# A fused attention, MLP and routed-expert kernel: the opening and the first block in another order

## What is computed

```python
# 1. linear attention with a decaying state: 4 sequences, 8 heads, 768 tokens, head size 48
for t in range(S):
    kt, vt, rt = (k[:, :, t], v[:, :, t], r[:, :, t])
    cur = np.einsum('bhd,bhe->bhde', u[None] * kt, vt)
    y[:, :, t] = np.einsum('bhd,bhde->bhe', rt, state + cur)
    state = w[None, :, :, None] * state + np.einsum('bhd,bhe->bhde', kt, vt)
# 2. dense MLP on x = y as 3072 rows of 384: w_in 384x2048, w_out 2048x384
h = np.maximum(x @ w_in, 0.0); x2 = h * h @ w_out
# 3. eight experts (384 -> 1024 -> 384) of 384 tokens each; a greedy assignment by sorted logits
out[mask] = np.maximum(x2[mask] @ w1[e], 0.0) @ w2[e]
```

## Time and profile before

| | |
|---|---|
| time, median of 3 executions | 803.26 us (802.25 to 804.04) |
| the profiled execution | 805.37 us |
| its span in the trace | 803.3 us |
| TensorE matmul busy | 785.6 us, 98% |
| VectorE busy | 537.0 us, 67% |
| ScalarE busy | 273.4 us, 34% |
| GpSimd busy | 175.8 us, 22% |

### The profile page before, as it was taken

One profiled execution on the slowest core, in us unless ns is written; L12 is line 12 of the kernel. 1 busy time (PEld: TensorE's weight loads), 2 busy tenths in 40 slices (PEclk: granted clock), 3 DMA queues, 4 the chain that ended last, 5 costly groups with the idle time before them and its releaser, 6 DMA issues.

```text
span 803.3 us, 16845 instructions
## 1 busy us (share of the span) xinstructions
PE 785.6 (98%) x6663; PEld 654.2 (81%) x6663; DVE 537.0 (67%) x1280; ACT 273.4 (34%) x511; POOL 175.8 (22%) x169
## 2 busy tenths in 40 slices
PE   8799999999999999999999999989999999999996
PEld 5677777777777877777777888668999999999996
DVE  7887767776677776777776545665867757667321
ACT  3443324433433343334434444311222122122321
POOL 5523142212222222222120040001122221231211
PEclk9999999999999999999999999999999999999999
DMA  8734225666666666666675566327467466564950
GB/s 265 247 135 135 83 95 184 224 214 207 200 208 215 206 205 220 214 214 221 214 260 170 173 215 212 137 70 287 163 229 262 169 224 218 222 250 144 341 218 29
DMA packets 62910, 158.72 MB, mean 198 GB/s; under 512 B 8304, under 2 KB 11632, under 8 KB 62832
## 3 DMA queue, kind: packets, MB, share of 16 engines
q1 hardware_dynamic: 56880, 144.28, 53.2%
q0 software_dynamic: 3072, 9.44, 3.6%
q10 hardware_dynamic: 2880, 3.93, 1.3%
HBM read 106.24 MB, written 51.38 MB: 196 GB/s over the span
## 4 chain that ended last, share of the span: by engine, by line
PE 90%; DMA 4%; DVE 2%; issue 1%; SPq 1%; ACT 0%; POOL 0%; POOLq 0%; DVEq 0%
PE ACC L1534 25%; PE U L1508 24%; PE ACC L1727 13%; PE U L1714 13%; DMA stage<-in_dw 3%; PE P L1625 3%; PE P L1391 3%; PE P L1408 2%; PE P L1478 2%; PE P L1400 1%; PE ACC L1571 1%; PE P L1490 1%; DMA WL<-split_low 1%; PE P L1650 1%; PE P L1452 0%
## 5 line engine op out<-in xcount | busy, mean ns | idle before, releaser
L1010 DVE TENSOR_TENSOR hr<-hr 128x512 f32<-128x512 f32 x96 | 67.9, 707 | 80.9 <-ACT hr L774 80.7
L1508 PE MATMUL U<-XH,WH 128*128 128x512 f32 x285 | 113.4, 398 | 0.0
L1508 PE MATMUL U<-XH,WL 128*128 128x512 f32 x285 | 112.9, 396 | 0.0
L1508 PE MATMUL U<-XL,WH 128*128 128x512 f32 x285 | 112.9, 396 | 0.0
L774 ACT ACTIVATE hr<-U 128x512 f32<-128x512 f32 x96 | 57.3, 596 | 162.0 <-PE U L1508 160.0
L1534 PE MATMUL ACC<-HH,WH 128*128 128x512 f32 x252 | 105.6, 419 | 2.7 <-DVE HL L1024 2.7
L1534 PE MATMUL ACC<-HL,WH 128*128 128x512 f32 x252 | 99.9, 397 | 0.0
L1534 PE MATMUL ACC<-HH,WL 128*128 128x512 f32 x252 | 99.8, 396 | 0.0
L1040 DVE TENSOR_TENSOR stage<-stage 128x512 fp32r<-128x512 f32 x80 | 68.8, 861 | 26.2 <-ACT stage L754 23.9
L886 ACT ACTIVATE HH<-U 128x384 fp32r<-128x384 f32 x64 | 31.5, 492 | 145.3 <-PE U L1714 142.3
L754 ACT ACTIVATE HH<-hr 128x512 fp32r<-128x512 f32 x84 | 53.1, 632 | 77.2 <-DVE hr L1010 77.2
(11 more groups left out here) (252 smaller groups left out, 1472.2 us busy)
## 6 DMA issues: line engine op xcount, KB each, us to landing
stage<-in_ew SPq DMA_DIRECT2D x80, 256.0 KB, 3.6
split_high<-stage SPq DMA_DIRECT2D x80, 256.0 KB, 2.1
split_low<-stage SPq DMA_DIRECT2D x80, 256.0 KB, 2.5
WH<-split_high SPq DMA_DIRECT2D x40, 512.0 KB, 5.9
WL<-split_low SPq DMA_DIRECT2D x40, 512.0 KB, 6.6
tok<-in_tok SPq DMA_DIRECT2D x24, 640.0 KB, 7.0
rk<-in_rk SPq DMA_DIRECT2D x22, 448.0 KB, 5.8
stage<-in_dw SPq DMA_DIRECT2D x8, 768.0 KB, 7.8
```

The lines of the kernel that those rows point to most:

```text
L1010: tt(hr[:, s % 2, :], hr[:, s % 2, :], hr[:, s % 2, :], ALU.mult).then_inc(sq_done, 1)
L1508: ins = mm(U[s % 2][:, :], w_up((WH, WL)[a], k, s), (XH, XL)[b][:, q, k, :], start=(n == 0), stop=(n == 3 * KT - 1))
```

## The change

Nothing is computed in another way and no instruction is added or taken out; the order changes in five places.

1. DVE, opening: the low part XL of sequence 0 and the masks of sequence 2 stand ahead of the scaling of sequence 3.
2. SP, opening: chunk 1 of the weights is asked for right behind the transposed rows of unit 4, ahead of its token rows.
3. POOL, opening: both products of sequences 2 and 3 stand ahead of the weighted keys of sequence 2.
4. ACT and DVE: chunk 1 is split at the end of the opening, ahead of the relu and the square of the first hidden tile, and no longer behind them.
5. PE, first block: the down tile of step 2 moves behind the up tile of step 3; the down tile of step 3 moves to step 4, where two down tiles follow each other.

```diff
@@ sync
             def opening_unit(b):
-                sp.wait_ge(at_mm, 2 * b + 2)
                 sp.wait_ge(y_mm, b + 1)
                 sp.wait_ge(st_mm, b + 1)
-                load_unit(BATCH + b, b, b)
+                load_tok(BATCH + b, b)
 
             sp.wait_ge(ld_stage[0], 16)
-            opening_unit(0)
+            sp.wait_ge(at_mm, 2)
+            load_rk(BATCH, 0)
             sp.wait_ge(at_mm, 2 * BATCH)
             load_weights(1)
+            opening_unit(0)
+            load_rk(BATCH + 1, 1)
             opening_unit(1)
@@ gpsimd
             pool.wait_ge(scaled, 1)
-            for b in range(BATCH):
-                unit(0, b, False)
+            for b in range(2):
+                products(0, b, True)
+                weighted(0, b, False)
+            for b in range(2, BATCH):
+                products(0, b, False)
+            for b in range(2, BATCH):
+                weighted(0, b, False)
             pool.wait_ge(tab, TAB_STEPS)
             with pool.Fori(1, NC) as c:
                 for b in range(BATCH):
-                    unit(c, b, True)
+                    products(c, b, False)
+                    weighted(c, b, True)
@@ scalar, block
                         nc.scalar.activation(hr[:, s % 2, :], U[s % 2][:, :], ACT.Relu).then_inc(relu_done, 1)
-                        if not post and s == 0:
-                            split_chunk(1)
@@ scalar, opening
                 if b == 1:
                     split_chunk(0)
+            split_chunk(1)
 
             blocks(act, body)
@@ vector, block
-                    if moe and not post and s == 0:
-                        split_chunk(1)
@@ vector, opening
             diagonal(0, 1)
+            task(0, 0, opening_out(0), "Y", 0)
+            opening_mask(2)
             opening_scale(3)
-            opening_mask(2)
-            task(0, 0, opening_out(0), "Y", 0)
             diagonal(0, 2)
...
             scale(1, 0)
+            split_chunk(1)
@@ tensor
                     if post or s > 0:
                         up(m, 1 - q, s)
+                    if moe and not post and s == LAG + 1:
+                        pe.wait_ge(wlo_done, 2)
+                        down(m, 0)
                     for n, kind, b in tasks_at(s, att, moe, post):
                         task(c, (att, moe, post), n, kind, b)
-                    if moe and not post and s >= LAG and (s - LAG) % GROUP == 0:
+                    if moe and not post and s > LAG and (s - LAG) % GROUP == 0:
                         pe.wait_ge(wlo_done, 2 * ((s - LAG) // GROUP) + 2)
...
-                    elif moe and (s >= LAG or post):
+                    elif moe and not post and s == 2 * LAG:
+                        down(m, 1)
+                        down(m, LAG)
+                    elif post or s > 2 * LAG:
                         down(m if s >= LAG else m - 1, (s - LAG) % NF1)
```

More of the change, by code:

```diff
@@ L654, in by_head, with products @@
                 return t.rearrange("p (h d) -> p h d", d=HDIM)
-            def unit(c, b, state):
+            def products(c, b, first):
                 u = BATCH * c + b
@@ L661, in unit @@
                 nc.gpsimd.tensor_tensor(r_t, r_t, k_t, ALU.mult).then_inc(rk_step, 1)
-                if not state:
+                if first:
                     pool.wait_ge(ld_urow, 16)
@@ L665, in unit, with weighted @@
                 nc.gpsimd.tensor_tensor(r_t, r_t, urow[:, :], ALU.mult).then_inc(rku_done, 1)
+            def weighted(c, b, state):
+                u = BATCH * c + b
+                k_t = tok[:, b, DM:2 * DM]
                 if not state:
```

## The result

The changed kernel takes 806.25 us (median of 7 runs, 803.83 to 808.01), the kernel before, in 7 runs beside it, 802.25 (801.30 to 804.04). The ratio is 1.0046 with an interval of 1.0027 to 1.0065: **slower**, by some 0.5%, where 801.0 had been forecast. The profiled execution has 808.01 us and a span of 806.2.

The account below looks back on a forecast made before the run. TensorE's waiting and slow clock around the first down tile were taken as the bound. 2.35 us won, 0.1 taken off, gave 2.2: 805.37 to 803.1 profiled, median 803.26 to 801.0, range 799.4 to 801.6 (chance 0.55).

Parts of the forecast that it names:

- What bounds the kernel: First block: TensorE's 2.7 us wait ahead of the first down tile plus 1.6 us of slow clock, 4.3 us at most.
- The clock's 1.6 us: First down tile and the up tile behind it: time lost to a lowered clock after TensorE stood still, 1.6 us.
- The same 2.2 off it gives 801.0: Whole kernel: the 2.2 us gain taken from the median of 803.26 us gives 801.0 us.
- Opening, masks ahead of the scaling: Opening on VectorE: masks run inside the load wait, TensorE ends the opening about 1.4 us earlier; costed at nothing.
- Chunk 1 at 30.5, token rows at 32.8: Opening's transfers: the weight chunk lands at 30.5 us, unit 4's token rows take its old place at 32.8.
- The diagonal at 36.4, blocked: VectorE, unit 4: the diagonal waits for GpSimd's two products, slowed by mutual blocking, until 36.4 us.
- the unblocked 34.9: VectorE, unit 4: start of the diagonal if VectorE and GpSimd do not block each other, 34.9 us.
- Split of chunk 2 ends at 45.1, up tile 4 with it: First block: VectorE's split ends at 45.1 us, before 43.96; up tile 4 waits 0.5 to 1 us for it.
- From up tile 4 to up tile 5, 7.6 us: TensorE, first block: 5.5 us plus a down tile of 2.10; up tile 5 starts at 52.7, 2.35 us won.
- The clock: "I expect no fall": First block: the long wait is cut into about 1.5 and 0.5 us, so the clock stays up; 1.6 us within 2.35.
- B: Rival: unit 4's token rows land late, near 36 us, and clock is lost in the open; 805.2 us, chance 0.12.
- A: Rival: VectorE's train eats the gain, TensorE waits for chunk 2 until 46 or later; 802.6 us, chance 0.27.

Follow-up runs that it names:

- the second trace: The kernel before, run and traced once more with nothing changed: 802.11 us, span 800.3.
- experiment 8's second kernel: The kernel before with only 24 unused products added in TensorE's wait at the first gathers: 803.30 us, ratio 1.0003.
- experiment 9: Changed kernel with unit 4's high and low parts made early and 24 unused products at the gathers, 804.00 us, beside the same with the old opening, 802.03 us.
- experiment 3: The changed kernel with TensorE's old order, so the opening's changes alone on the kernel before: 805.80 us, ratio 1.0024.
- experiment 7's first kernel: The kernel before with only chunk 1 asked for ahead of the token rows and split early: 803.35 us, ratio 1.0001.
- experiment 7's second kernel: The kernel before with only the opening's new order of VectorE's masks and GpSimd's products: 803.87 us, ratio 1.0018.
- experiment 9's first trace: Trace of the changed kernel with unit 4's high and low parts made early and 24 unused products at the gathers: 804.00 us, ratio 1.0011.

## Why the prediction was wrong, step by step

*What bounds the kernel.* Right as a reading of one execution, wrong as a yardstick. The clock's 1.6 us and 1.1 us of the wait belonged to the profiled execution and not to every one: the second trace has neither. Nor is it rare: experiment 8's second kernel, which is before up to the gathers, had the wait of 2.7 us and the fall again. "The same 2.2 off it gives 801.0" took from the median what the median does not hold. The profiled execution lay 2.1 us above the median; that this might sit in just the place under study was the warning.

*Opening, masks ahead of the scaling: costed at nothing.* TensorE was earlier, and it was worth nothing, as said: in the part with masks and GpSimd alone the wait ahead of the down tile was 2.9 us against 1.6 in the second trace of before. VectorE gained 0.5 us only (split of chunk 0 at 24.88; 25.40 in that trace). But the opening as a whole costs: about 2 us by experiment 9. The prediction did follow rows, products and diagonal, and put the diagonal at 36.4; it did not set that against before, where masks could start at 35.0 (second trace), since its yardstick had them at 36.44. Which part it is stays open: 0.1 us for transfers with splits and 1.4 us (0.2 to 2.7) for masks with GpSimd make up the 1.9 us (0.4 to 3.5) of experiment 3 only within their intervals, all by ratios.

*Chunk 1 at 30.5, token rows at 32.8.* Earlier: ScalarE's split began at 29.23, GpSimd's product at 32.44. In other traces of the changed opening VectorE's split began anywhere from 29.9 to 33.6; one landing time was the wrong thing to forecast.

*The diagonal at 36.4, blocked.* It started at 35.10, near the unblocked 34.9. The square started 0.02 us ahead of the product (32.42 and 32.44) and kept its 0.68 us; it was the product that lost, 1.54 us instead of 1.0. VectorE was blocked later: the square at 37.37, beside a product that began at 36.80, took 1.50. That it blocks was right, where was wrong. The Trainium skill's rule, page "SBUF — State Buffer", section "Who interferes with whom", that of the two engines the second to start is blocked, agrees with both squares.

*Split of chunk 2 ends at 45.1, up tile 4 with it.* 44.00, and 44.05: right in kind, 1.1 us better.

*From up tile 4 to up tile 5, 7.6 us.* **This is the step that failed**: 13.3. Its own work was right (7.84), but it added durations of tiles and asked of no instruction in it whether it was released. The wait for XL, 2.26 us, was priced at nothing. A program printed with its waits shows `xlo_done` on that row; the question to ask was when XL is made, and the trace of before has it.

*The clock: "I expect no fall".* Wrong in both traces of the changed kernel, 3.2 us in the first. It followed from the step above in the first; in the second it fell behind three small waits, 1.1, 0.7 and 0.4 us, where waits of 0.6, 1.1 and 0.7 had brought no fall in the first.

*The rivals.* None was it. B, slower through late token rows, named the right side and nearly the right time (805.2) by the wrong way: the rows landed in order, at 32.44 and not near 36. Its link, late rows that hold products, diagonal and masks, is nevertheless what the opening's cost runs through. A, VectorE's train, has its share in that cost; its slack was put at 1.8 us, but from 45.1 to 45.9 it is 0.8.

By ratios the parts then go together so, in us of 803: TensorE's new order with its wait cured -0.8 (0.9990); the wait, and the clock behind it, +2.4 on the new opening (1.0046 less 1.0016) and +3.3 on the old one (1.0031 less 0.9990); the opening +1.7 (experiment 9). That makes 3.3 to 4.2 us over before; measured are 3.7, with an interval of 2.2 to 5.2. Each term has an interval of over 1 us to either side, so the sum agrees but does not test the terms.

## What to carry to other kernels

An instruction that moves forward meets waits that were always there and cost nothing. For each one ask which semaphores it waits for, buffers that it reuses above all, and when the trace of before shows them set; adding up durations will not find them. A transfer that is asked for earlier makes the one that it passes later: ask what waits for that one too. Work put ahead of ready work because its transfer comes earlier holds that ready work until the landing, which wandered here by 3.7 us. And before a saving is read from one profile, compare its time with the median: what only some executions lose can be won in those alone.

## What the hardware showed that I had not expected

The length of a wait alone does not decide whether the clock falls. Behind 1.6 to 1.7 us at the gathers it fell in 4 of 12 traces. At the first down tile it fell behind 1.9 us (experiment 7's first kernel), behind 2.7 us (the first profile of before and experiment 8's second kernel) and behind 4.1 us (experiment 3), and not behind 1.6 us (the second trace of before) nor behind 2.9 us (experiment 7's second kernel). What decides is open here. What a fall costs at the gathers was alike, 1.5 to 1.8 us. With the wait filled it came there in none of four traces, which chance alone would give once in five times, (8/12)^4.

Either engine can be held through several instructions of the other. GpSimd's product of 128x384, 1.02 us at 35.03, took 4.35 us at 43.45, beside five VectorE instructions in a row (42.25 to 46.94); it ended at 47.80, 0.86 us behind the last of them, as if it had hardly begun before. A little later in the same trace it is VectorE:

```profile
49.28 1.33 POOL L679 TENSOR_TENSOR Sd<-S,w 112x384 f32<-112x384 f32 x1 [1.49 <-DVE S L974]
50.58 0.99 POOL L663 TENSOR_TENSOR tok<-tok 128x384 f32<-128x384 f32 x1
...
49.84 3.34 DVE L950 TENSOR_TENSOR WL<-stage,WH 128x1536 fp32r<-128x1536 f32 x1
```

The split of 1.75 us took 3.34, and ended 1.6 us behind the second of GpSimd's two instructions. By the page of the Trainium skill named above the second to start waits for the first; here the one that began beside a running instruction got no turn at four changes of instruction on VectorE, and none at one on GpSimd. It is not always so: in experiment 9's first trace the product that began at 33.26, beside a split that ran to 34.73, was done at 35.60, so it had its turn when the split ended, and the square behind the split (1.51 us) was the one that waited. What decides between the two is open.
